# One-hot compares by groups of four chunks, and no unread gather, in a fused attention, expert and gating kernel

## The chip, the cores and the metric

The kernel runs on one core of a Trainium2 chip. The metric is the device time of one execution in microseconds; less is better. Three executions of the kernel before are shown, with one profiled execution among them.

## What is computed

Three layers in a row, all in float32, for 2 batches of 768 tokens with 384 features. First a linear attention with decay, 8 heads of 48. Then a mixture of 8 experts, in which each token goes to one expert, and last a gating layer with a spatial mix. The part around the change is the choice of the expert and the sorting of tokens by expert:

```python
for b in range(B):
    prev_e = -1
    for s in range(S):
        fresh_e = int(np.argmax(logits[b, s]))
        if s == 0 or local_gate[b, s] < 0.5:
            e = fresh_e
        else:
            e = prev_e if prev_e >= 0 else fresh_e
        prev_e = e
        ...
        h = np.maximum(x[b, s] @ w1[e], 0.0)
        out[b, s] = p[e] * (h @ w2[e])
```

The third layer takes relu(x @ w_in), halves it into u and v, normalises v over its features, mixes it over the tokens with w_spatial and a bias, multiplies with u and applies w_out.

## The kernel before, in words

The 1536 tokens are NC = 12 chunks of P = 128, a token on each partition. The kernel has one program for each engine, and the order of the work is written out by hand in each; they meet by semaphores alone. Three stages follow each other, with only weight loads and their splitting running across the borders.

*Attention* (to about 82 us). For each chunk TensorE multiplies, VectorE scales and masks (`mask`, L665, and `decay`, L657), GpSimd makes the bonus products, and ScalarE stores each pair of chunks of x to `x_dram` (`store_rows`, semaphore `s_xd`). Row 0 of `x_dram` is zero, token n is row n + 1. The router's logits of each chunk are made at L1206.

*Routing* (to about 98 us). VectorE computes, in some twenty small steps, `slot_i`: for each token its place in a list sorted by expert, where expert e has room for 1536 places. It is split by bits: `lo_i` (the last seven bits, the place within a block of 128) and `hi_i` (the block). `spread` (L762) is 1 where block `hi_i` is one of 16 blocks, the first two of each expert, and `spread_r` (L767) is `spread` times the token's row number. `place` (L771) is, for each chunk c, a 128 x 128 matrix with a 1 where `lo_i` of the token equals the column number from `iota_w`. The product of `place` and `spread_r`, summed over the twelve chunks in `bank[4]` (L1250), is the list of row numbers: column 2e + t holds the 128 rows that expert e takes in its half t. VectorE copies it to `inv` (L774, semaphore `s_inv`), and GpSimd gathers with it from `x_dram` into `x_in` (`gather_x`, L574, two indirect DMAs for each expert, their semaphores `s_xin`). TensorE transposes what has landed (`transpose_x`, L1264), ScalarE makes the high part `xT_h` (L1033), VectorE the low part `xT_l` (L794), and the first expert matmul (L1256) can start. Between its steps TensorE runs filler matmuls (`stay_warm`, L1129), whose results nobody reads.

The `place` compares are twelve instructions on VectorE, one for each chunk, each with its own step of `s_place`; the twelve matmuls on TensorE each wait for theirs. A compare of that form takes its scalar from a float32 column, which is `lo_f`, a cast of `lo_i` (L761). `Chain.link` makes an engine wait for the instruction it wraps.

GpSimd, after the attention, waits for all rows of x and for the zero row, clears `row_0` (L581), issues an indirect DMA by it (L582) that reads row 0 of `x_dram` 128 times into the tile `one_hot`, and then waits for `s_inv`. Its data is not used; its semaphore `s_unread` is waited for only in the body that handles experts with more than 256 tokens, before `one_hot` is written there.

*Experts and gating.* For each expert 96 matmuls with 256 columns, then 48 with 384; weights arrive as float32 in `raw`, and ScalarE and VectorE split them into a high and a low part (L394, L399). Between the last expert and the gating stage come the tests for overflow blocks, and the gathers of y.

The change also bears on where tiles lie: they are placed one behind the other, in steps of 32 bytes per partition, so tiles behind two that go move down.

Of the kernel before, what the change touches and what calls it, by code (L numbers as in the profile page):

```python
# [9 lines left out]
U32 = mybir.dt.uint32  # L10
ALU = mybir.AluOpType
# [3 lines left out]
P = 128  # L15
B, H, S, DH = 2, 8, 768, 48
D = H * DH
# [4 lines left out]
NC = B * NCB  # L22
# [29 lines left out]
def build(nc, r_feat, k_feat, r_tok, k_tok, v_tok, w_feat, u_tok, w_route, w1, w2, w_in, w_spT, b_sp, w_out, out):  # L52
    x_dram = nc.dram_tensor("x_dram", (NTOK + 1, D), F32).ap()
# [7 lines left out]
    with ExitStack() as ctx:  # L61
        taken = [0]

        def sb(name, shape, dt=F32, scope=ctx):
            size = 2 if dt == BF16 else 4
            for n in shape[1:]:
                size *= n
            taken[0] += -(-size // 32) * 32
            return scope.enter_context(nc.sbuf_tensor(name, shape, dt))

        def sem(name):
            return ctx.enter_context(nc.semaphore(name))
# [18 lines left out]
        iota_w = sb("iota_w", [P, BLK])  # L91
        one_hot = sb("one_hot", [P, 2, BLK])
# [22 lines left out]
        upto = sb("upto", [P, E, NC])  # L115
        row_of = sb("row_of", [P, E, NC])
        lo_i = sb("lo_i", [P, NC], I32)
        lo_f = sb("lo_f", [P, NC])
        row_0 = sb("row_0", [P, 1], U32)
        hi_i = sb("hi_i", [P, NC], I32)  # L120
        col_no = sb("col_no", [P, 2 * E])
        token = sb("token", [P, NC])
# [51 lines left out]
        place = sb("place", [P, NC, P], F32R, scope=att)  # L174
# [111 lines left out]
        s_place = sem("s_place")  # L286
        s_inv_p = sem("s_inv_p")
        s_inv = sem("s_inv")
        s_unread = sem("s_unread")
        s_meta = sem("s_meta")  # L290


# [87 lines left out]
        def raw_as(q, k):  # L380
            return raws[q][:, :].rearrange("p (k m) -> p k m", k=k)
# [111 lines left out]
        def _(pool):  # L493
            chain = Chain(pool, s_pool)
# [27 lines left out]
            for n in range(NC):  # L522
                p, q = divmod(n, 2)
# [48 lines left out]
            def gather_x(e):  # L572
                for t in range(2):
# [3 lines left out]

            pool.wait_ge(s_xd, 16 * NI)
            pool.wait_ge(s_zrow, 32)

            chain.link(nc.gpsimd.memset(row_0[:, :], 0))  # L581
            nc.gpsimd.indirect_dma_start(out=one_hot[:, :, :].rearrange("p a j -> p (a j)")[:, 0:D], out_offset=None,  # L582
                                         in_=x_dram, in_offset=bass.IndirectOffsetOnAxis(ap=row_0[:, 0:1], axis=0))\
                .then_inc(s_unread, 16)
            pool.wait_ge(s_inv, 1)
            gather_x(0)
            for e in range(1, E):
# [34 lines left out]
        def _(dve):  # L622
            chain = Chain(dve, s_dve)
# [101 lines left out]
            def per_e(ap):  # L725
# [32 lines left out]
                                               ALU.max))  # L758
            nc.vector.tensor_scalar(hi_i[:, :], slot_i[:, :], -P, None, ALU.bitwise_and)
            chain.link(nc.vector.tensor_scalar(lo_i[:, :], slot_i[:, :], P - 1, None, ALU.bitwise_and))  # L760
            nc.vector.tensor_copy(lo_f[:, :], lo_i[:, :])  # L761
            chain.link(nc.vector.tensor_tensor(spread[:, :, :],  # L762
                                               hi_i[:, :].rearrange("p (c a) -> p c a", a=1)
                                               .to_broadcast([P, NC, 2 * E]),
# [2 lines left out]
            nc.vector.tensor_tensor(spread_r[:, :, :], spread[:, :, :],  # L767
                                    token[:, :].rearrange("p (c a) -> p c a", a=1).to_broadcast([P, NC, 2 * E]),
                                    ALU.mult)
            for c in range(NC):  # L770
                nc.vector.tensor_scalar(place[:, c, :], iota_w[:, 0:P], lo_f[:, c:c + 1], None, ALU.is_equal)\  # L771
                    .then_inc(s_place, 1)
            dve.wait_ge(s_inv_p, 1)
            nc.vector.tensor_copy(inv[:, :], bank[4][:, 0:2 * E]).then_inc(s_inv, 1)  # L774
            nc.vector.tensor_copy(slot_f[:, :], slot_i[:, :])
# [106 lines left out]
            with dve.If(last >= 1):  # L882
                with dve.Fori(1, NOV + 1) as i:
                    with dve.If(i <= last):
                        dve.wait_ge(o_raw, i * 64)
                        for q, (high, low) in enumerate(((w1_h[:, :, 0:FH], w1_l[:, :, 0:FH]),
                                                         (w1_h[:, :, FH:F], w1_l[:, :, FH:F]),
                                                         (w2_h[:, 0:KF // 2, :], w2_l[:, 0:KF // 2, :]),
                                                         (w2_h[:, KF // 2:KF, :], w2_l[:, KF // 2:KF, :]))):
                            raw = raw_as(q, high.shape[1])  # L890
                            nc.vector.tensor_copy(high, raw).then_inc(o_split, 1)
                            dve.wait_ge(o_split, (i - 1) * 8 + (2 * q + 1))
                            nc.vector.tensor_tensor(low, raw, high.bitcast(F32), ALU.subtract).then_inc(o_split, 1)
                        dve.wait_ge(s_unread, 16)
                        nc.vector.tensor_tensor(rel[:, :], slot_f[:, :], ov_base[:, bass.ds(i - 1, 1)]
                                                .to_broadcast([P, NC]), ALU.subtract).then_inc(o_rel, 1)
                        dve.wait_ge(o_rel, i)
                        for c in range(NC):
                            if c >= 2:
                                dve.wait_ge(o_take, (i - 1) * NC + (c - 1))  # L900
                            nc.vector.tensor_scalar(one_hot[:, c % 2, :], iota_w[:, :], rel[:, c:c + 1], None,
                                                    ALU.is_equal).then_inc(o_hot, 1)
                        dve.wait_ge(o_take, i * NC)
                        for k in range(KD):
                            nc.vector.tensor_copy(xT_h[:, k, :], bank[5 + k][:, 0:BLK]).then_inc(o_xh, 1)
                        dve.wait_ge(o_xh, i * KD)
                        for k in range(KD):
                            nc.vector.tensor_tensor(xT_l[:, k, :], bank[5 + k][:, 0:BLK], xT_h[:, k, :].bitcast(F32),
                                                    ALU.subtract).then_inc(o_xl, 1)
                        for fp in range(4):  # L910
                            k = slice(2 * fp, 2 * fp + 2)
                            high = hT_h[:, k, :].rearrange("p k t -> p (k t)")
                            dve.wait_ge(o_up, (i - 1) * 4 + (fp + 1))
                            nc.vector.tensor_scalar(high, bank[fp][:, :], 0.0, None, ALU.max).then_inc(o_hh, 1)
                            dve.wait_ge(o_hh, (i - 1) * 4 + (fp + 1))
                            nc.vector.scalar_tensor_tensor(hT_l[:, k, :].rearrange("p k t -> p (k t)"), bank[fp][:, :], 0.0,
                                                           high.bitcast(F32), ALU.max, ALU.subtract).then_inc(o_hl, 1)
                        dve.wait_ge(o_yout, i * 32)
                        for t in range(2):
                            dve.wait_ge(o_down, (i - 1) * 2 + (t + 1))  # L920
                            nc.vector.tensor_copy(y_out[:, t, :], bank[4 + t][:, 0:D]).then_inc(o_yev, 1)
# [201 lines left out]
        def _(pe):  # L1123
# [122 lines left out]
            mm(bank[2][:, 0:E * NC], later_b[:, :], hot_v, start=False, stop=True).then_inc(s_count, 1)  # L1246
            stay_warm(11, ident[:, :])
            for c in range(NC):
                pe.wait_ge(s_place, c + 1)
                done = mm(bank[4][:, 0:2 * E], place[:, c, :], spread_r[:, c, :], start=(c == 0), stop=(c == NC - 1))  # L1250
            done.then_inc(s_inv_p, 1)
            pe.wait_ge(s_bbc, 16)
# [202 lines left out]
```

## Time and profile before

| | us |
|---|---|
| three executions | 382.17, 384.67, 390.24 |
| median | 384.67 |
| profiled execution, own time | 384.67 |
| profiled execution, span | 382.9 |
| mean granted TensorE clock, share of full | 0.987 |

The span runs from the first to the last instruction of the profiled execution; its own time holds 1.8 us more around it. Full clock is 2.4 GHz. In the rows, PE is TensorE's matmuls, PEld its weight loads, DVE VectorE, ACT ScalarE, POOL GpSimd, and SPq the queue of the engine that issues most DMAs. L12 is line 12 of the kernel before. `<-` behind an idle time names what ended it.

### The profile page before, as it was taken

How to read it: one execution, taken by the hardware profiler on the slowest of the kernel's cores; microseconds unless marked ns; L12 is line 12 of the kernel's file. 1: busy time of each engine (PE TensorE's matmuls, PEld its weight loads, DVE VectorE, ACT ScalarE, POOL GpSimd, SP SyncE). 2: the span in 40 equal slices, each digit the busy share in tenths (PEclk: the TensorE clock that was granted, in tenths of full speed). 3: DMA queues.
4: the chain of work that ended last, by engine and by line, in shares of the span. 5: the costliest groups of instructions: out<-in, count | busy, mean ns of one | idle time of the engine just before them, and what ended most of it. 6: DMA issues, size and time to landing. Idle time of an engine off the chain costs nothing.

```text
span 382.9 us, 6205 instructions
## 1 busy us (share of the span) xinstructions
PE 364.2 (95%) x2515; PEld 348.8 (91%) x2515; DVE 224.0 (59%) x389; ACT 141.7 (37%) x216; POOL 105.4 (28%) x123
## 2 busy tenths in 40 slices
PE   5899999999799999999999999499999999999996
PEld 5799899986799999999999999278999998899996
DVE  6799689638684958687484955048035605605530
ACT  1023233322364645557272434047411326621122
POOL 2697999612110203031010000515700002500000
PEclk9999999999899999999999999699999999999999
DMA  6989989821595767869594510500310020000002
GB/s 225 409 307 353 388 342 325 300 84 53 166 334 176 237 242 253 299 211 348 182 308 162 184 43 21 145 2 3 89 37 0 0 99 26 2 0 2 0 29 95
DMA packets 30863, 61.97 MB, mean 162 GB/s; under 512 B 2433, under 2 KB 17794, under 8 KB 30834
## 3 DMA queue, kind: packets, MB, share of 16 engines
q1 hardware_dynamic: 23762, 48.00, 35.4%
q10 hardware_dynamic: 5216, 7.87, 5.7%
q0 software_dynamic: 1856, 5.70, 4.8%
q8 instruction: 21, 0.34, 0.4%
q14 instruction: 8, 0.07, 0.1%
HBM read 51.53 MB, written 10.03 MB: 161 GB/s over the span
## 4 chain that ended last, share of the span: by engine, by line
PE 91%; DMA 3%; DVE 2%; issue 2%; SPq 1%; ACT 1%; POOL 0%; DVEq 0%
PE bank L1256 23%; PE bank L1258 23%; PE bank L1257 23%; PE bank L1183 6%; PE bank L1140 3%; PE bank L1179 2%; PE bank L1163 2%; DMA vN<-v_tok 2%; PE bank L1206 2%; PE bank L1153 1%; PE bank L1264 1%; PE bank L1129 1%; PE bank L1196 1%; PE bank L1352 1%; DMA x_in<-x_dram,inv 1%
## 5 line engine op out<-in xcount | busy, mean ns | idle before, releaser
L1256 PE MATMUL bank<-xT_h,w_h 128*128 128x256 f32 x192 | 55.0, 287 | 1.6 <-DVE xT_l L794 1.6
L399 DVE TENSOR_TENSOR w_l<-raw,w_h 128x1536 fp32r<-128x1536 f32 x29 | 50.4, 1758 | 10.2 <-ACT w_h L394 10.2
L1258 PE MATMUL bank<-xT_h,w_l 128*128 128x256 f32 x192 | 55.0, 287 | 0.0
L1257 PE MATMUL bank<-xT_l,w_h 128*128 128x256 f32 x192 | 55.0, 287 | 0.0
L394 ACT ACTIVATE w_h<-raw 128x1536 fp32r<-128x1536 f32 x32 | 46.9, 1485 | 12.3 <-DVE inv L774 8.0
L574 POOL DMA_INDIRECT x_in<-x_dram,inv x16 | 19.0, 1187 | 96.1 <-PE bank L1264 86.8
L1256 PE MATMUL bank<-w_h,hT_h 128*128 128x384 f32 x128 | 43.4, 339 | 0.0
L1258 PE MATMUL bank<-w_h,hT_l 128*128 128x384 f32 x128 | 42.8, 334 | 0.0
L1257 PE MATMUL bank<-w_l,hT_h 128*128 128x384 f32 x128 | 42.8, 334 | 0.0
L1038 ACT ACTIVATE hT_h<-bank 128x512 fp32r<-128x512 f32 x32 | 19.0, 594 | 59.5 <-PE bank L1258 59.5
L1256 PEld LDWEIGHTS bank<-xT_h,w_h 128*128 128x128 f32 x192 | 37.5, 195 | 1.9 <-DVE xT_l L794 1.9
L1258 PEld LDWEIGHTS bank<-xT_h,w_l 128*128 128x128 f32 x192 | 37.6, 196 | 0.0
L1257 PEld LDWEIGHTS bank<-xT_l,w_h 128*128 128x128 f32 x192 | 37.5, 195 | 0.0
L608 POOL TENSOR_TENSOR v_l<-v_nrm,v_h 128x512 fp32r<-128x512 f32 x12 | 15.5, 1292 | 64.9 <-ACT v_h L1096 64.9
L857 DVE SCALAR_TENSOR_TENSOR hT_l<-bank,hT_h 128x512 fp32r<-128x512 f32 x32 | 21.8, 686 | 17.7 <-ACT hT_h L1038 17.7
L1258 PE MATMUL bank<-w_sp_h,v_l 128*128 128x384 f32 x96 | 32.1, 334 | 0.0
L1256 PE MATMUL bank<-w_sp_h,v_h 128*128 128x384 f32 x96 | 32.1, 334 | 0.0
L1257 PE MATMUL bank<-w_sp_l,v_h 128*128 128x384 f32 x96 | 32.1, 334 | 0.0
L959 DVE TENSOR_TENSOR gate_in<-bank,b_bc 128x384 f32<-128x384 f32 x16 | 8.9, 558 | 35.4 <-PE bank L1258 35.4
L1183 PE MATMUL bank<-vN,scores 128*128 128x96 f32 x192 | 28.2, 275 | 0.0
L1183 PEld LDWEIGHTS bank<-vN,scores 128*128 128x128 f32 x192 | 24.8, 192 | 0.0
L1105 ACT ACTIVATE g_h<-gated 128x384 fp32r<-128x384 f32 x16 | 8.4, 527 | 42.9 <-DVE gated L963 42.9
(194 smaller groups left out, 812.3 us busy)
## 6 DMA issues: line engine op xcount, KB each, us to landing
raw<-w SPq DMA_DIRECT2D x28, 768.0 KB
vN<-v_tok SPq DMA_DIRECT2D x6, 576.0 KB, 6.6
rT<-r_feat SPq DMA_DIRECT2D x6, 512.0 KB, 7.2
kT<-k_feat SPq DMA_DIRECT2D x6, 512.0 KB, 8.3
kN<-k_tok SPq DMA_DIRECT2D x6, 512.0 KB, 8.6
raw<-w ACTq DMA_DIRECT2D x4, 768.0 KB
y_dram<-y_out SPq DMA_DIRECT2D x16, 192.0 KB, 1.9
rN<-r_tok SPq DMA_DIRECT2D x6, 384.0 KB, 7.1
```

The costliest lines, as they stand in the source:

```text
L394: nc.scalar.activation(parts[n][3], raw_of(n), ACT.Copy).then_inc(s_high, 1)
L399: eng.tensor_tensor(low, raw_of(n), high.bitcast(F32), ALU.subtract).then_inc(s_low[kind], 1)
L574: nc.gpsimd.indirect_dma_start(out=x_in[:, t, :], out_offset=None, in_=x_dram, in_offset=bass.IndirectOffsetOnAxis(ap=inv[:, 2 * e + t:2 * ...
L608: nc.gpsimd.tensor_tensor(v_l[:, c, :], v_nrm[q][:, :], v_h[:, c, :].bitcast(F32), ALU.subtract).then_inc(g_vl, 1)
L857: nc.vector.scalar_tensor_tensor(hT_l[:, k, :].rearrange("p k t -> p (k t)"), bank[fp][:, :], 0.0, hT_h[:, k, :].rearrange("p k t -> p (k ...
L959: nc.vector.tensor_tensor(gate_in[q][:, :], bank[3 + f][:, 0:HALF], b_bc[:, t * HALF:(t + 1) * HALF], ALU.add).then_inc(g_sin, 1)
L1038: nc.scalar.activation(hT_h[:, 2 * fp:2 * fp + 2, :].rearrange("p k t -> p (k t)"), bank[fp][:, :], ACT.Relu).then_inc(s_hh, 1)
L1140: done = mm(bank[2 * q + head % 2][:, m * CH:(m + 1) * CH], k_dec[q][rows, m, :], r_dec[n % 3][rows, m, :], start=True, stop=True)
L1183: done = mm(bank[4 + q][:, at:at + 2 * DH], scores[q][:, g * NP + m, :], vN[:, p % 2, q, m, g * DH:(g + 2) * DH], start=first_one, stop=Tr ...
L1256: mm(dst, left_h, right_h, start=(k == 0), stop=False)
L1257: mm(dst, left_h, right_l, start=False, stop=False)
L1258: return mm(dst, left_l, right_h, start=False, stop=(k == last_k))
```

## The change

The twelve compares that write `place` become three, each for four chunks, in a form with two tensor inputs: `lo_i` (int32), repeated along the columns, against `iota_w`, repeated along the chunks. Each of the three raises `s_place` by one, and TensorE waits once for each four matmuls. `lo_f` is no longer made. Beside that, the gather into `one_hot` that nobody reads goes, with `row_0`, its semaphore and the wait for it. Two tiles go, of 64 and 32 bytes per partition with rounding.

```diff
--- before.py
+++ after.py
@@ -115,8 +115,6 @@
         upto = sb("upto", [P, E, NC])
         row_of = sb("row_of", [P, E, NC])
         lo_i = sb("lo_i", [P, NC], I32)
-        lo_f = sb("lo_f", [P, NC])
-        row_0 = sb("row_0", [P, 1], U32)
         hi_i = sb("hi_i", [P, NC], I32)
         col_no = sb("col_no", [P, 2 * E])
         token = sb("token", [P, NC])
@@ -286,7 +284,6 @@
         s_place = sem("s_place")
         s_inv_p = sem("s_inv_p")
         s_inv = sem("s_inv")
-        s_unread = sem("s_unread")
         s_meta = sem("s_meta")
 
 
@@ -577,11 +574,6 @@
 
             pool.wait_ge(s_xd, 16 * NI)
             pool.wait_ge(s_zrow, 32)
-
-            chain.link(nc.gpsimd.memset(row_0[:, :], 0))
-            nc.gpsimd.indirect_dma_start(out=one_hot[:, :, :].rearrange("p a j -> p (a j)")[:, 0:D], out_offset=None,
-                                         in_=x_dram, in_offset=bass.IndirectOffsetOnAxis(ap=row_0[:, 0:1], axis=0))\
-                .then_inc(s_unread, 16)
             pool.wait_ge(s_inv, 1)
             gather_x(0)
             for e in range(1, E):
@@ -758,7 +750,6 @@
                                                ALU.max))
             nc.vector.tensor_scalar(hi_i[:, :], slot_i[:, :], -P, None, ALU.bitwise_and)
             chain.link(nc.vector.tensor_scalar(lo_i[:, :], slot_i[:, :], P - 1, None, ALU.bitwise_and))
-            nc.vector.tensor_copy(lo_f[:, :], lo_i[:, :])
             chain.link(nc.vector.tensor_tensor(spread[:, :, :],
                                                hi_i[:, :].rearrange("p (c a) -> p c a", a=1)
                                                .to_broadcast([P, NC, 2 * E]),
@@ -767,9 +758,12 @@
             nc.vector.tensor_tensor(spread_r[:, :, :], spread[:, :, :],
                                     token[:, :].rearrange("p (c a) -> p c a", a=1).to_broadcast([P, NC, 2 * E]),
                                     ALU.mult)
-            for c in range(NC):
-                nc.vector.tensor_scalar(place[:, c, :], iota_w[:, 0:P], lo_f[:, c:c + 1], None, ALU.is_equal)\
-                    .then_inc(s_place, 1)
+            for g in range(3):
+                c = slice(g * NC // 3, (g + 1) * NC // 3)
+                nc.vector.tensor_tensor(place[:, c, :], lo_i[:, c].rearrange("p (c a) -> p c a", a=1)
+                                        .to_broadcast([P, NC // 3, P]),
+                                        iota_w[:, 0:P].rearrange("p (a j) -> p a j", a=1)
+                                        .to_broadcast([P, NC // 3, P]), ALU.is_equal).then_inc(s_place, 1)
             dve.wait_ge(s_inv_p, 1)
             nc.vector.tensor_copy(inv[:, :], bank[4][:, 0:2 * E]).then_inc(s_inv, 1)
             nc.vector.tensor_copy(slot_f[:, :], slot_i[:, :])
@@ -891,7 +885,6 @@
                             nc.vector.tensor_copy(high, raw).then_inc(o_split, 1)
                             dve.wait_ge(o_split, (i - 1) * 8 + (2 * q + 1))
                             nc.vector.tensor_tensor(low, raw, high.bitcast(F32), ALU.subtract).then_inc(o_split, 1)
-                        dve.wait_ge(s_unread, 16)
                         nc.vector.tensor_tensor(rel[:, :], slot_f[:, :], ov_base[:, bass.ds(i - 1, 1)]
                                                 .to_broadcast([P, NC]), ALU.subtract).then_inc(o_rel, 1)
                         dve.wait_ge(o_rel, i)
@@ -1246,7 +1239,8 @@
             mm(bank[2][:, 0:E * NC], later_b[:, :], hot_v, start=False, stop=True).then_inc(s_count, 1)
             stay_warm(11, ident[:, :])
             for c in range(NC):
-                pe.wait_ge(s_place, c + 1)
+                if c % (NC // 3) == 0:
+                    pe.wait_ge(s_place, 3 * c // NC + 1)
                 done = mm(bank[4][:, 0:2 * E], place[:, c, :], spread_r[:, c, :], start=(c == 0), stop=(c == NC - 1))
             done.then_inc(s_inv_p, 1)
             pe.wait_ge(s_bbc, 16)
```

## Rows read from the trace of the kernel before

**Rows 1.** The page: busy time of TensorE; the chain that ended last, by engine.

```profile
PE 364.2 (95%) x2515; PEld 348.8 (91%) x2515; DVE 224.0 (59%) x389; ACT 141.7 (37%) x216; POOL 105.4 (28%) x123
...
PE 91%; DMA 3%; DVE 2%; issue 2%; SPq 1%; ACT 1%; POOL 0%; DVEq 0%
```

**Rows 2.** The chain of waits, 88 to 99 us: start, length, what.

```profile
89.13 2.45 PE bank L1250 x12
...
93.39 3.06 DMA x_in<-x_dram,inv
...
98.69 0.39 PE bank L1256
```

**Rows 3.** Timeline of all engines, 88 to 92 us: start, length, instruction, count.

```profile
88.05 0.17 DVE L761 CAST lo_f<-lo_i 128x12 f32<-128x12 int32 x1
88.13 0.35 DVE L762 TENSOR_TENSOR spread<-hi_i,col_no 128x192 f32<-128x192 int32 x1
...
88.79 2.43 DVE L771 TENSOR_SCALAR place<-iota_w,lo_f 128x128 fp32r<-128x128 f32 x12
89.13 2.34 PEld L1250 LDWEIGHTS bank<-spread_r,place 128*128 128x128 f32 x12 [0.46 <-DVE place L771]
```

**Rows 4.** VectorE by line and shape: count, busy us, mean ns, idle before.

```profile
L665 DVE TENSOR_TENSOR scores<-bank,later 128x512 f32<-128x512 f32 x24 | 15.3, 678 | 0.2 <-PE bank L1140 0.2
L657 DVE TENSOR_TENSOR k_dec<-kT,tab_k 128x512 f32<-128x512 f32 x12 | 11.6, 965 | 0.9 <-DMA kT<-k_feat 0.8
...
L771 DVE TENSOR_SCALAR place<-iota_w,lo_f 128x128 fp32r<-128x128 f32 x12 | 2.4, 279 | 0.0
...
L762 DVE TENSOR_TENSOR spread<-hi_i,col_no 128x192 f32<-128x192 int32 x1 | 0.4, 351 | 0.0
```

**Rows 5.** Timeline of TensorE: the router at 80.8, the first expert at 100 and 104.

```profile
80.83 0.84 PE L1206 MATMUL bank<-w_rt,xT_att 128*128 128x9 f32 x6
...
99.99 0.42 PE L1256 MATMUL bank<-xT_h,w_h 128*128 128x256 f32 x1
100.21 0.41 PE L1257 MATMUL bank<-xT_l,w_h 128*128 128x256 f32 x1
...
104.00 0.28 PE L1257 MATMUL bank<-xT_l,w_h 128*128 128x256 f32 x1
104.12 0.28 PE L1258 MATMUL bank<-xT_h,w_l 128*128 128x256 f32 x1
```

**Rows 6.** Timeline of GpSimd, 83 to 94 us.

```profile
83.98 1.17 POOL L582 DMA_INDIRECT one_hot<-x_dram,row  x1 [0.30 <-POOL row L581]
92.05 1.04 POOL L574 DMA_INDIRECT x_in<-x_dram,inv  x1 [6.89 <-DVE inv L774]
```

**Rows 7.** Lines L574, L946 and L1250: durations in ns, min/median/max.

```profile
L574 POOL DMA_INDIRECT x_in<-x_dram,inv x16: 944/948/2468, 92.0 to 199.3; - x16
...
L946 DVE TENSOR_SCALAR v_nrm<-v_act,mean_var,std x12: 545/578/777, 255.9 to 332.2; 128x512 f32<-128x512 f32 x12
...
L1250 PE MATMUL bank<-spread_r,place x12: 277/277/278, 89.1 to 91.3; 128*128 128x16 f32 x12
```

**Rows 8.** DMA issues: count and us from issue to landing.

```profile
one_hot<-x_dram,row POOLq DMA_INDIRECT x1, 3.9
```

**Rows 9.** Stretches: length, busy us of each engine, granted clock, DMA share, GB/s.

```profile
8.00:12.00 4.00, 1.75 (x20) 1.39 (x20) 3.57 (x7) 0.60 (x1) 1.03 (x2) 1.00 1.03 423
86.00:88.00 2.00, 1.92 (x18) 1.93 (x19) 1.61 (x8) 0.00 (x0) 0.00 (x0) 1.00 0.32 85
96.00:99.00 3.00, 0.86 (x5) 0.62 (x6) 1.39 (x3) 0.87 (x2) 1.37 (x2) 1.00 0.05 9
99.00:104.00 5.00, 5.00 (x31) 5.00 (x30) 3.73 (x3) 1.84 (x2) 0.52 (x1) 0.66 0.68 199
243.00:250.00 7.00, 4.33 (x8) 2.16 (x9) 0.00 (x0) 0.00 (x0) 3.34 (x4) 0.51 0.51 148
```

**Rows 10.** Timeline between the experts and the gating stage.

```profile
245.68 3.78 PE L1129 MATMUL bank<-b_bc,ident 128*128 128x512 f32 x4 [4.97 <-issue]
```

## Prediction

> **What bounds the kernel now.** I read the page first: TensorE is busy in 95% of the span; the chain that ended last runs over it for 91% [rows 1]. The sum can therefore change only where TensorE has nothing useful to do. The edited lines lie in one such place, between the router and the first expert. There the chain of waits, in order of time, is the second view [rows 2]: VectorE builds `lo_i`, `lo_f`, `spread` and `spread_r` one by one, twelve compares write `place`, twelve matmuls at L1250 turn it into the list of rows, VectorE copies that to `inv`, GpSimd issues two gathers, the second one's landing releases the transposes, ScalarE and VectorE split them, and the first expert matmul starts at 98.69; its long pieces are the rows shown. Everything in this chain is serial, so a microsecond here is a microsecond of the span. The reader is to see in [rows 2, 3, 6] that the gathers with their issues (92.05 to 96.45) are longer than the whole piece that is rewritten (88.05 to 91.58).
>
> The profiled execution took 384.67 us, of which 382.9 is the span and 1.8 lies around it; it is also the median of the three runs shown (382.17 to 390.24), so a sum against it is a sum against the median.
>
> **Part 1: `lo_f` goes.** The cast starts at 88.05 and the next instruction already at 88.13 [rows 3]: VectorE lets the following one in 0.08 us later, and the link behind it waited for `spread`, not for the cast. Gain 0.08.
>
> **Part 2: twelve compares become three.** Before, the first `place` starts at 88.79, and twelve take 2.43 us in all at 279 ns each [rows 3, 4]: (2.43 - 0.28)/11 = 0.195 from start to start, an overlap of 0.084. The new form has two tensor inputs and 4x128 = 512 outputs. The row of its size is the mask, 128x512 with a broadcast operand, 678 ns [rows 4]; `spread`, with an int32 input and two broadcasts, lies no higher: 351 ns for 192 elements, so 0.155 + 1.02 ns an element through both rows. GpSimd is idle from 85.15 to 92.05 [rows 6], so the long cases of the same size, `k_dec` at 965 ns, which run beside GpSimd work, are only the upper bound. With the same overlap of 0.084 the three end at 88.71 + 2 x 0.594 + 0.678 = 90.58. Before, the last ends at 88.79 + 2.43 = 91.22. So VectorE is done 0.64 earlier. By the upper bound (965 ns) they would end at 88.71 + 2 x 0.881 + 0.965 = 91.44, 0.22 later than now.
>
> One rule speaks against this step. A one-input operation with per-partition scalars takes at least 545 ns for 512 elements [rows 7], against 279 for 128, which is 0.69 ns for each further element; two-input ones take the 1.02 [rows 4]. The Trainium skill, "VectorE: DVE Perf Modes", section "Mode 2×_2P — use both read ports for one tensor", says that fp32 tensor_scalar may run at two results a cycle while tensor_tensor stays at one. By that rule alone, at 0.96 GHz, the old form would be 12 x 0.067 = 0.80 us of elements and the new 1.60, and the edit would lose 0.80; the trace agrees with its direction, but shows that at 128 elements the fixed part of each instruction is larger than what the rule saves.
>
> **The tail on TensorE.** This is where I choose. Today each matmul at L1250 follows its own compare: the first load starts at 89.13, 0.06 after its compare ended, and the last matmul ends at 91.58, 0.36 after the last compare [rows 2, 3]. After the change four matmuls are released together by the last compare, at 90.58 + 0.06 = 90.64. How fast four 128x128 loads with 16 moving columns follow each other isn't in the trace, because VectorE paces them. Bounds: no faster than all at once; no slower than today's pace, (2.45 - 0.277)/11 = 0.198 [rows 2, 7]. Nearest is the router's matmul, also a 128x128 load with few columns: six in 0.84 us, (0.84 - 0.277)/5 = 0.113 apart if one takes as long [rows 5]. I take it, the more so as the expert's matmuls load a fresh 128x128 every 0.12 us [rows 5]. The last one ends at 90.64 + 0.277 + 3 x 0.113 = 91.26; before, 91.58. Gain of parts 1 and 2 together: 0.32 us. With no time between them it is 91.58 - 90.92 = 0.66, with 0.198 it is 0.07; with the slow 965 ns compares and 0.113 it becomes a loss of 0.54. TensorE's first release moves to 88.71 + 0.678 + 0.06 = 89.45 from 89.13.
>
> **Part 3: the unread gather goes.** The gather takes 1.17 us up to 85.15, and GpSimd then idles 6.89 us until `inv` [rows 6]. Its data moves alone: 85 GB/s in 86 to 88 [rows 9], which is 0.17 MB of its 0.20. So its time costs nothing now and its removal gives nothing. What it may have bought is that the first useful gather isn't the first of its kind. Issue: 1.17 against 1.04 for the next one, and a median of 0.948 for all sixteen [rows 6, 7]: +0.13 on the path if that is a first-use cost. Landing: 3.9 us [rows 8] against 3.06 for the one on the path [rows 2], 0.84 longer. I book only the 0.13: the transposes' split waits for both gathers, the second is issued 1.34 us after the first, so a first landing 0.84 late still lands ahead of the second one. Bounds: -0.13 (the issue at 92.05 gets shorter instead, as the median is by 0.09, plus some rounding) and +0.97 (0.13 + 0.84, if the second is held up too).
>
> **The rest.** The wait on `s_unread` and its users stand in the body for overflow blocks; between the experts and the fillers of the gating stage TensorE sits idle for 4.97 us up to 245.68 [rows 10], so no matmul of that body runs. Nothing gained. The tiles behind `lo_f` and `row_0` move down by 96 bytes. At the start, transfers into them reach 423 GB/s with the 16 DMA engines full [rows 9]; there is little to win by another address. Zero, at most 0.1 us either way. Nine fewer waits of TensorE cost nothing, it waits for the same compares.
>
> Sum: 384.67 - 0.32 + 0.13 = 384.48, say **384.5 us**.
>
> **The rivals.** *A cold gather on the path.* The missing first use shows in the landing of the second gather too: 384.48 + 0.84 = 385.3. For it: the only long landing at a quiet time is the very first. Against: that gather read one row 128 times, which may be slow by itself, and the one on the path took 3.06.
>
> *The clock.* While it waits for the gather, TensorE does 0.86 us of work in 3, and soon after, the granted clock falls: 0.66 on average in 99 to 104 [rows 9], which is 2 x 0.34 x 5 = 3.4 us at 1.2 GHz. Matmuls then start 0.22 apart instead of 0.12 [rows 5], so these 3.4 us hold 15.5 instead of 28.3, a loss of 12.8 x 0.12 = 1.5 us. A shift of some tenths may make the fall vanish: 384.48 - 1.5 = 383.0. The Trainium skill, "TensorE: Matmul & The Clock Gate", section "What's actually happening", says that the gate's watch isn't reset when a kernel starts; by that, one trace can't tell whether the next execution has this fall; no run here shows it yet, and it weighs on both signs.
>
> *Slower than before: the two together.* The first real gather bears all of the first use (+0.97), TensorE idles nearly a microsecond longer before the first expert, and the clock stays at 1.2 GHz for a second stretch as long as the first (+1.5): 384.67 - 0.32 + 0.97 + 1.5 = 386.8. Its place is L574 to L1256 at 92 to 104; it decides once the wait behind the transposes and the split exceeds today's by enough for the fall to come before 98.7. For it: around the 4.97 us gap that ends at 245.68 the clock is at half for 7 us (0.51 in 243 to 250) [rows 9, 10]. Against: the issue cost seen is 0.13 only.
>
> *TensorE was the pace.* The loads of L1250 lie end to end (12 in 2.34 us, [rows 3]) with one recorded idle. If they can't go faster than 0.198, the twelve start at 89.45 and end at 91.90, 0.32 later than now: 384.67 + 0.32 + 0.13 = 385.1. Against: 0.12 at the expert's loads.
>
> **How the numbers follow.** Forecast 0.45; cold gather 0.15; clock fall gone 0.12; both together 0.13; TensorE's pace 0.10; anything outside these 0.05. All terms are far below 2% (7.7 us), about what a measurement of this kernel can tell from no change. The cases reach from 383.0 to 386.8; three executions of one and the same kernel lay 2.5 under and 5.6 over their median, so I add 1.2 below and 0.8 above for the median: 381.8 to 387.6. Over 2% faster has no mechanism (0.01); over 2% slower needs a first-use cost several times what the rows show (0.04); within 2%: 0.95.
>
> **What would show it.** Three `place` rows of about 0.68 us starting near 88.7 to 89.9 on this time scale; L1250 in groups of four, the last ending 0.3 earlier against `spread_r`; the first x_in issue at about 1.17 and the second landing some 3.1 us after its issue; no `one_hot` transfer. The forecast is wrong if the issue or landing of the first gathers grows by over a microsecond, if the compares take near 1 us, or if the stretch at 1.2 GHz is absent or doubled; then the matching rival holds. If none of these shows and the time is off all the same, it comes from a stage that I hold to be untouched.

## The result: 1.2% slower, and the profile after

| | before | changed |
|---|---|---|
| six executions each, median, us | 384.68 | 388.88 |
| lowest and highest, us | 382.17, 390.24 | 387.37, 390.41 |
| ratio, 95% interval | | 1.012 [1.0077, 1.0165] |
| profiled execution: own time, span, us | 384.67, 382.9 | 386.37, 384.6 |
| twelve executions beside 29 of before, later, median, us | 384.65 | 387.06 |
| ratio there, 95% interval | | 1.0063 [1.0027, 1.0099] |

The ratios leave out executions more than 1.5% above the fastest of their kernel; medians and mean clocks are over all, unless said otherwise. The loss is within the 2% that I called no change, but clear of noise. The first median lies outside my range of 381.8 to 387.6, the later one of 387.06 just inside it. Between the two profiled executions the difference is only 1.7 us; the changed kernel's was one of its quicker ones.

The page of the changed kernel shows the same picture as [rows 1], a little lower on TensorE:

```profile
PE 362.9 (94%) x2515; PEld 347.6 (90%) x2515; DVE 224.4 (58%) x379; ACT 141.6 (37%) x216; POOL 105.2 (27%) x121
...
PE 90%; DMA 3%; DVE 2%; issue 2%; SPq 1%; ACT 1%; POOL 0%; DVEq 0%; POOLq 0%
```

The chain of waits, which answers to [rows 2]: start, length, what.

```profile
91.42 0.19 DVE inv L768
...
91.68 0.82 issue
92.50 1.18 POOL x_in L571
...
93.98 3.99 DMA x_in<-x_dram,inv
...
100.20 0.58 PE bank L1250
```

From the start of `inv` to the first expert matmul it was 98.69 - 91.60 = 7.09 us before (`inv` began at 91.60 there) and is 100.20 - 91.42 = 8.78 now. The 1.69 us more are three pieces: the first gather starts 1.08 behind the start of `inv` instead of 0.45 (+0.63; the 0.82 "issue" is time in which GpSimd waited for nothing that the profile shows), it takes 1.18 instead of 1.04 (+0.14), and the second gather lands 3.99 behind its start instead of 3.06 (+0.93).

The timeline of the changed kernel shows the third piece, and the compares; it answers to [rows 3] and [rows 6].

```profile
88.83 1.89 DVE L763 TENSOR_TENSOR place<-lo_i,iota_w 128x512 fp32r<-128x512 int32 x3
...
89.57 1.82 PE L1244 MATMUL bank<-spread_r,place 128*128 128x16 f32 x12 [0.59 <-DVE place L763]
...
92.50 1.18 POOL L571 DMA_INDIRECT x_in<-x_dram,inv  x1 [18.57 <-DVE inv L768]
...
93.22 1.76 DVE L396 TENSOR_TENSOR w_l<-raw,w_h 128x1536 fp32r<-128x1536 f32 x1 [0.30 <-ACT w_h L391]
...
93.98 1.83 POOL L571 DMA_INDIRECT x_in<-x_dram,inv  x1 [0.30 <-issue]
```

The second gather's issue (the time in which GpSimd executes the instruction that starts the transfer) takes 1.83 us, 0.88 more than before. What differs is who was first. Line L396 is VectorE's low part of expert 1's first weights. Before, it and the second gather both started at 93.39. Now it starts at 93.22, the gather at 93.98, and the gather's issue ends at 95.81, 0.83 us after the VectorE instruction has ended at 94.98.

The new compares, which answer to [rows 4]: three, 684 ns each.

```profile
L763 DVE TENSOR_TENSOR place<-lo_i,iota_w 128x512 fp32r<-128x512 int32 x3 | 1.9, 684 | 0.0
```

And the stretches of [rows 9]: no transfer in 86 to 88; the clock falls to the same mean in 99 to 104, now with less work in that stretch, since the first expert starts 1.5 later.

```profile
86.00:88.00 2.00, 1.88 (x18) 1.81 (x18) 1.61 (x8) 0.00 (x0) 0.00 (x0) 1.00 0.00 0
99.00:104.00 5.00, 3.80 (x20) 3.80 (x21) 4.42 (x4) 0.49 (x3) 1.73 (x2) 0.66 0.46 100
243.00:250.00 7.00, 3.05 (x4) 1.41 (x5) 0.00 (x0) 0.00 (x0) 4.42 (x5) 0.76 0.69 193
```

### The profile page after: what moved, and what is told of

Read it like the earlier page. It is cut to its first block, busy times and chain, and to the rows that moved or that the text cites. A ratio compares the mean times of both kernels' runs of the same rounds, so it can differ in the third digit from the quotient of the medians.

```text
span 384.6 us, 6193 instructions
## 1 busy us (share of the span) xinstructions
PE 362.9 (94%) x2515; PEld 347.6 (90%) x2515; DVE 224.4 (58%) x379; ACT 141.6 (37%) x216; POOL 105.2 (27%) x121
## 4 chain that ended last, share of the span: by engine, by line
PE 90%; DMA 3%; DVE 2%; issue 2%; SPq 1%; ACT 1%; POOL 0%; DVEq 0%; POOLq 0%
PE bank L1250 23%; PE bank L1252 23%; PE bank L1251 23%; PE bank L1176 6%; PE bank L1133 3%; PE bank L1172 2%; PE bank L1156 2%; DMA vN<-v_tok 2%; PE bank L1199 2%; PE bank L1146 1%; PE bank L1258 1%; PE bank L1189 1%; PE bank L1122 1%; DMA x_in<-x_dram,inv 1%; PE bank L1346 1%
## 5 line engine op out<-in xcount | busy, mean ns | idle before, releaser
L1250 PE MATMUL bank<-xT_h,w_h 128*128 128x256 f32 x192 | 55.1, 287 | 1.6 <-DVE xT_l L788 1.6
L396 DVE TENSOR_TENSOR w_l<-raw,w_h 128x1536 fp32r<-128x1536 f32 x29 | 50.4, 1756 | 9.8 <-ACT w_h L391 9.0
L571 POOL DMA_INDIRECT x_in<-x_dram,inv x16 | 19.8, 1237 | 107.9 <-PE bank L1258 86.9
L1250 PE MATMUL bank<-w_h,hT_h 128*128 128x384 f32 x128 | 43.4, 339 | 0.0
L1250 PEld LDWEIGHTS bank<-xT_h,w_h 128*128 128x128 f32 x192 | 37.4, 195 | 1.9 <-DVE xT_l L788 1.9
L1250 PE MATMUL bank<-w_sp_h,v_h 128*128 128x384 f32 x96 | 32.1, 334 | 0.0
```

Source lines behind the costliest of these rows:

```text
L396: eng.tensor_tensor(low, raw_of(n), high.bitcast(F32), ALU.subtract).then_inc(s_low[kind], 1)
L571: nc.gpsimd.indirect_dma_start(out=x_in[:, t, :], out_offset=None, in_=x_dram, in_offset=bass.IndirectOffsetOnAxis(ap=inv[:, 2 * e + t:2 * ...
L1250: mm(dst, left_h, right_h, start=(k == 0), stop=False)
```

## The experiments

The question was which of the three edits costs, and then what stands behind each of the three pieces. No kernel leaves out a part of the computation. "Behind `inv`" is counted from the start of the copy to `inv`, unless I say from its end (0.17 to 0.19 us later), as my expectations did.

**compares_only.** The changed kernel with the gather put back (here and below, the tile, the semaphore and the wait for it in the overflow body come back with it, and are not shown):

```diff
             pool.wait_ge(s_zrow, 32)
+            chain.link(nc.gpsimd.memset(row_0[:, :], 0))
+            nc.gpsimd.indirect_dma_start(out=one_hot[:, :, :].rearrange("p a j -> p (a j)")[:, 0:D], out_offset=None,
+                                         in_=x_dram, in_offset=bass.IndirectOffsetOnAxis(ap=row_0[:, 0:1], axis=0))\
+                .then_inc(s_unread, 16)
             pool.wait_ge(s_inv, 1)
```

> The changed kernel with the unread gather put back: only the compares differ from the kernel before (and 64 bytes of tiles). Theory (the removed gather is what costs): ratio to before at or just under 1, 0.998 to 1.001, some 0.3 us faster, first expert matmul about 7.1 us after inv. Rival (the compares, or their gap on TensorE, cost): ratio 1.008 to 1.016 as in the changed kernel.

Measured: ratio 0.9988 [0.9947, 1.0029]. Its timeline: the first gather 0.45 behind `inv`, the second not held up though VectorE's instruction started 0.02 earlier, first expert matmul 7.16 behind `inv`. Neither the compares nor TensorE's wider gap ahead of the first `place` cost anything that this comparison, good to 0.4%, can see.

```profile
86.08 1.21 POOL L581 DMA_INDIRECT one_hot<-x_dram,row  x1 [0.30 <-POOL row L580]
...
96.74 0.17 DVE L775 CAST inv<-bank 128x16 uint32<-128x16 f32 x1 [1.72 <-PE bank L1252]
...
97.19 1.05 POOL L573 DMA_INDIRECT x_in<-x_dram,inv  x1 [9.90 <-DVE inv L775]
...
98.53 1.81 DVE L398 TENSOR_TENSOR w_l<-raw,w_h 128x1536 fp32r<-128x1536 f32 x1 [0.30 <-ACT w_h L393]
98.55 0.95 POOL L573 DMA_INDIRECT x_in<-x_dram,inv  x1 [0.31 <-issue]
...
103.90 0.38 PE L1258 MATMUL bank<-xT_h,w_h 128*128 128x256 f32 x1 [1.64 <-DVE xT_l L795]
```

**gather_gone_only.** The kernel before, with its twelve compares and all tiles in place, without the gather:

```diff
-            chain.link(nc.gpsimd.memset(row_0[:, :], 0))
-            nc.gpsimd.indirect_dma_start(out=one_hot[:, :, :].rearrange("p a j -> p (a j)")[:, 0:D], out_offset=None,
-                                         in_=x_dram, in_offset=bass.IndirectOffsetOnAxis(ap=row_0[:, 0:1], axis=0))\
-                .then_inc(s_unread, 16)
...
-                        dve.wait_ge(s_unread, 16)
```

> The kernel before without the unread gather, tiles left where they are: the twelve compares stay. Theory: ratio 1.008 to 1.016, first x_in issue over 0.8 us after inv, the second issue near 1.8 us, landing near 4.0, first expert matmul 8.5 to 9 us after inv. Rival (compares or tile addresses): ratio 0.998 to 1.003.

Measured: 1.0074 [1.0034, 1.0113], just under the expected range. The whole pattern is back: 1.08, 1.18, 1.83, and 8.66 to the first expert matmul. The removed gather is the loss; the tiles' addresses aren't.

```profile
91.53 0.17 DVE L770 CAST inv<-bank 128x16 uint32<-128x16 f32 x1 [0.37 <-PE bank L1245]
...
92.61 1.18 POOL L574 DMA_INDIRECT x_in<-x_dram,inv  x1 [18.86 <-DVE inv L770]
...
93.33 1.76 DVE L399 TENSOR_TENSOR w_l<-raw,w_h 128x1536 fp32r<-128x1536 f32 x1 [0.30 <-ACT w_h L394]
...
94.09 1.83 POOL L574 DMA_INDIRECT x_in<-x_dram,inv  x1 [0.30 <-issue]
...
100.19 0.57 PE L1251 MATMUL bank<-xT_h,w_h 128*128 128x256 f32 x1 [1.64 <-DVE xT_l L790]
```

**gather_early.** The changed kernel with an unread gather of rows of `w_out` among the attention work:

```diff
+                if n == 2:
+                    chain.link(nc.gpsimd.memset(row_0[:, :], 0))
+                    nc.gpsimd.indirect_dma_start(..., in_=w_out, ...).then_inc(s_unread, 16)
```

> The changed kernel with a gather that nobody reads put among GpSimd's attention work at about 20 us (rows of w_out, by a zero index), some 70 us of other GpSimd work and waiting ahead of the first useful one. If the cost is a first use alone (code or rings made ready once), it is gone: ratio 0.997 to 1.003, first x_in issue 0.3 us after inv. If it is the pause or the other work since the last gather, it stays: ratio 1.007 to 1.016, and first matmul 8.5 us or more after inv.

Measured in only six executions: 1.0199 [1.0111, 1.0288], an interval that lies on both sides of 2%, and worse than either expectation. Why it is that much isn't shown. Its profile has `inv` at 94.16, but the changed kernel itself has it at 91.42 in one execution and at 94.59 in another (changed_again), so that says nothing of the edit. The time as a whole can't be read for the question; the timeline of GpSimd can:

```profile
30.86 1.17 POOL L573 DMA_INDIRECT one_hot<-w_out,row  x1 [0.30 <-POOL row L572]
...
95.13 0.98 POOL L580 DMA_INDIRECT x_in<-x_dram,inv  x1 [18.53 <-DVE inv L777]
96.42 2.11 POOL L580 DMA_INDIRECT x_in<-x_dram,inv  x1 [0.30 <-issue]
```

The first useful gather still starts 0.97 behind `inv`, so a first use long ago doesn't cure the late start. But its own length is 0.98, not 1.18, and now the early one has the 1.17: 0.2 us belong to the first gather of a program, whenever it comes.

**plain_dma_warm.** A plain DMA in the gather's place:

```diff
+            nc.gpsimd.dma_start(one_hot[:, :, :].rearrange("p a j -> p (a j)")[:, 0:D], x_dram[1:P + 1, :])\
+                .then_inc(s_unread, 16)
             pool.wait_ge(s_inv, 1)
```

> The changed kernel with a plain GpSimd DMA of 128 rows of x_dram in the place of the unread gather. If GpSimd's DMA queue or rings must be made ready, this does it too: ratio 0.997 to 1.003. If it is the indirect instruction's own code, nothing is won: ratio 1.007 to 1.016 and the issue of the first x_in gather as late as in the changed kernel (0.9 us after inv). In between: landing back to 3.1 us, but the late issue stays, some 0.7 us of the 1.7.

Measured: 1.0049 [1.001, 1.0088], between the two.

```profile
83.35 0.79 POOL L580 DMA_DIRECT2D one_hot<-x_dram  x1 [9.49 <-DMA x_dram<-X]
...
91.36 0.18 DVE L773 CAST inv<-bank 128x16 uint32<-128x16 f32 x1 [0.70 <-PE bank L1250]
...
91.83 1.12 POOL L573 DMA_INDIRECT x_in<-x_dram,inv  x1 [7.69 <-DVE inv L773]
...
93.15 1.76 DVE L398 TENSOR_TENSOR w_l<-raw,w_h 128x1536 fp32r<-128x1536 f32 x1 [0.30 <-ACT w_h L393]
93.25 2.49 POOL L573 DMA_INDIRECT x_in<-x_dram,inv  x1 [0.30 <-issue]
```

The first gather starts 0.47 behind `inv`: the late start is cured, and not by an indirect DMA. Yet the first expert matmul comes 9.00 behind `inv`, later than in the changed kernel, because the second gather starts only 0.10 us behind VectorE's instruction and is held for 2.49 us, to 0.83 after its end (94.91). My "in between" case had the parts the wrong way round: start cured, landing not.

**low_after_move.** The changed kernel, one order changed on VectorE:

```diff
-            make_low(dve, first[1])
             move_x(0)
+            make_low(dve, first[1])
```

> The changed kernel with one order changed on VectorE: the low part of expert 1's first weights (make_low of first[1]) comes behind the move of x for expert 0, not ahead of it. Theory (the second gather's issue is held up by the VectorE instruction that started 0.8 us before it, a port that both need): the second issue falls from 1.83 to 0.95 us, its landing stays near 3.0 us behind its start, the first expert matmul comes 0.9 us earlier after inv (8.78 to 7.9), ratio 1.002 to 1.008, some 0.9 us under the changed kernel. Rival (the second issue is long because GpSimd's code or rings are cold): it stays at 1.8 and the time stays or rises.

Measured: 1.001 [0.9972, 1.0047]. The second issue is 0.96 us, the first expert matmul 7.92 behind `inv` instead of 8.78, as expected, while the late start (1.07) and the 1.18 stay. The ratio is a little better than the 1.002 to 1.008 that I had expected. The moved instruction now meets the first gather for expert 2, whose issue takes 2.25 us at 111.99; the ratio holds whatever that costs.

```profile
94.24 0.17 DVE L768 CAST inv<-bank 128x16 uint32<-128x16 f32 x1 [0.70 <-PE bank L1244]
...
95.31 1.18 POOL L571 DMA_INDIRECT x_in<-x_dram,inv  x1 [19.51 <-DVE inv L768]
...
96.80 0.96 POOL L571 DMA_INDIRECT x_in<-x_dram,inv  x1 [0.30 <-issue]
...
102.16 0.39 PE L1250 MATMUL bank<-xT_h,w_h 128*128 128x256 f32 x1 [1.71 <-DVE xT_l L788]
```

Over all kernels of this study the second gather's issue reads:

| kernel | VectorE's start ahead of the second gather's | its issue | ends after VectorE's end |
|---|---|---|---|
| before | 0.00 | 0.95 | not held |
| compares_only | 0.02 | 0.95 | not held |
| kept_filled | 0.01 | 0.95 | not held |
| plain_dma_warm | 0.10 | 2.49 | 0.83 |
| gather_before_wait | 0.45 | 2.12 | 0.81 |
| gather_early | 0.47 | 2.11 | 0.82 |
| changed, memset_in_place, fill_the_wait, gather_gone_only, changed_again | 0.74 to 0.76 | 1.82 to 1.85 | 0.82 to 0.83 |

The Trainium skill, "SBUF — State Buffer", section "SBUF: two separate sides", says that VectorE and GpSimd share a port pair, and that a VectorE operation with two SBUF inputs contends for it with a GpSimd operation that reads SBUF: whichever starts first has it for the whole instruction, and the other is blocked. The table agrees: a gather that is later by 0.10 us or more waits to the end. What it shows beyond this is that an indirect DMA's issue behaves like such an operation, and ends some 0.8 us behind the release.

Other places in the traces sharpen it. The three long issues further on in the kernel before fit too; the longest is the first pair of rows. A short instruction with two SBUF inputs does the same: `hit` (L782), 0.32 us long, started 0.11 ahead of the first useful gather of [rows 6], which ended 0.83 behind its end. So the 1.04 there is an issue of 0.95 with a short hold in it. The last pair is the counter-case: `hT_l` reads one of its inputs from PSUM (the tile `bank`), and a gather that starts within it isn't held.

```profile
146.38 1.76 DVE L399 TENSOR_TENSOR w_in_l<-raw,w_in_h 128x1536 fp32r<-128x1536 f32 x1 [1.16 <-ACT w_in_h L394]
146.49 2.47 POOL L574 DMA_INDIRECT x_in<-x_dram,inv  x1 [0.30 <-issue]
...
91.94 0.32 DVE L782 TENSOR_TENSOR hit<-expd,hot 128x96 f32<-128x96 f32 x1
...
162.49 0.68 DVE L857 SCALAR_TENSOR_TENSOR hT_l<-bank,hT_h 128x512 fp32r<-128x512 f32 x1
162.85 0.95 POOL L574 DMA_INDIRECT x_in<-x_dram,inv  x1 [13.89 <-PE bank L1264]
```

Over the 14 traces together, 61 gathers started 0.07 us or more behind a VectorE split of weights (L399 before), and all 61 ended 0.82 to 0.83 behind its end; 14 started 0.00 to 0.03 behind one, and none was held. Of 113 that started within an `hT_l` or `xT_l`, both with an input in PSUM, none took over 0.95.

**memset_in_place.** Only the memset where the gather was.

```diff
             pool.wait_ge(s_zrow, 32)
+            chain.link(nc.gpsimd.memset(row_0[:, :], 0))
             pool.wait_ge(s_inv, 1)
```

> The changed kernel with only the 128x1 memset where the unread gather was. If the late start of the first gather (0.89 us after inv, 0.29 before) comes from GpSimd having executed nothing for 18 us, a memset at 83.6 us cures it as any instruction would: start 0.3 us after inv. If it comes from the DMA-issuing code not having been used lately: start stays 0.85 to 0.95 us after inv. The issue stays at 1.18 and the second at 1.8 either way.

Measured in a single execution: 388.07 us, and in the timeline the start is 1.05 behind `inv` (0.88 from its end). Executing something isn't enough.

```profile
84.92 0.10 POOL L580 MEMSET row<- 128x1 uint32 x1 [9.64 <-DMA x_dram<-X]
...
92.81 0.17 DVE L772 CAST inv<-bank 128x16 uint32<-128x16 f32 x1 [0.70 <-PE bank L1248]
...
93.86 1.18 POOL L573 DMA_INDIRECT x_in<-x_dram,inv  x1 [8.84 <-DVE inv L772]
```

**gather_before_wait.** The unread gather (of `w_out`) ahead of the wait for the rows of x:

```diff
+            chain.link(nc.gpsimd.memset(row_0[:, :], 0))
+            nc.gpsimd.indirect_dma_start(..., in_=w_out, ...).then_inc(s_unread, 16)
             pool.wait_ge(s_xd, 16 * NI)
```

> The changed kernel with an unread gather (of w_out, by a zero index) as GpSimd's next work behind its last attention product, at about 74 us, ahead of its wait for the rows of x; then GpSimd idles some 17 us. If the late start of the first useful gather comes from other work having been done in between (as behind the early gather at 30 us), it is cured here: start 0.45 us after inv has begun, as before, issue 1.04. If it is the length of the idle time, it stays at 0.9 to 1.1. The second issue is 0.95 or about 2.4 in the first case, by whether it meets the VectorE instruction, and 1.8 in the second.

Measured in a single execution: 388.04 us.

```profile
76.71 1.18 POOL L579 DMA_INDIRECT one_hot<-w_out,row  x1 [0.30 <-POOL row L578]
...
93.57 0.17 DVE L775 CAST inv<-bank 128x16 uint32<-128x16 f32 x1 [0.70 <-PE bank L1252]
...
94.55 0.96 POOL L573 DMA_INDIRECT x_in<-x_dram,inv  x1 [16.66 <-DVE inv L775]
...
95.36 1.76 DVE L398 TENSOR_TENSOR w_l<-raw,w_h 128x1536 fp32r<-128x1536 f32 x1 [0.30 <-ACT w_h L393]
...
95.81 2.12 POOL L573 DMA_INDIRECT x_in<-x_dram,inv  x1 [0.30 <-issue]
```

No other work lies between this gather and the useful one, only 16.66 us of idle time, and the start is late, 0.98 behind `inv`. The second issue isn't the 1.8 that I expected with a late start: the first gather starts 0.10 earlier than in the changed kernel and its issue is 0.2 shorter, so the second starts only 0.45 behind VectorE and takes 2.12. In compares_only 9.90 us of idle time lay between the two and the start was 0.45.

So an earlier DMA issue of GpSimd cures the late start where a memset doesn't, but not from here. Idle time by itself does no harm up to 15.4 us. In the kernel before, the gather for expert 3 waits 15.41 us for the transposes and starts 0.27 behind their end at 127.35. The first gather of that kernel starts 0.28 behind the end of `inv`, that of the changed kernel 0.90.

```profile
126.53 0.82 PE L1264 MATMUL bank<-ident,x_in 128*128 128x128 f32 x6
...
127.62 1.74 POOL L574 DMA_INDIRECT x_in<-x_dram,inv  x1 [15.41 <-PE bank L1264]
```

If it is idle time, the effect is lost between 15.4 and 16.7 us. If it is what GpSimd's program has between the two gathers (here the waits for x and the zero row, there one wait), it has no such edge. No run separates these two.

**fill_the_wait.** The changed kernel with filler matmuls:

```diff
+            stay_warm(1, b_bc[:, 0:256])
...
+                    if e == 0 and t == 0:
+                        stay_warm(3, b_bc[:, 0:256])
                 done.then_inc(s_xt, 1)
+                if e == 0:
+                    stay_warm(3, b_bc[:, 0:256])
```

> The changed kernel with filler matmuls (128x256) in TensorE's waits for the gathers and for the split: one before the first landing, three between the two landings, three behind the transposes. They write a bank that nobody reads. Theory (part of the loss, 1 us or more, is the clock that falls because the wait has grown): granted clock stays at full through 100 to 104, mean clock of the runs up by some 0.004, ratio 1.001 to 1.007. Rival (the loss is the delay alone): ratio stays 1.008 to 1.012 or rises, as the fillers can only be in the way.

Measured: 1.0047 [1.001, 1.0084], first expert matmul 8.75 behind `inv`. The clock is at full in 99 to 104 (first row), but that doesn't show the fillers at work. In this execution `inv` starts only at 94.92, and the clock had fallen before it, to 0.79 in 82 to 98. The changed kernel without fillers has the same pattern in the profile of changed_again (second and third row):

```profile
99.00:104.00 5.00, 4.02 (x20) 3.01 (x21) 1.41 (x3) 0.87 (x2) 1.69 (x3) 1.00 0.17 44
...
82.00:98.00 16.00, 15.28 (x86) 11.65 (x86) 9.76 (x35) 4.16 (x7) 2.03 (x2) 0.79 0.11 32
...
99.00:104.00 5.00, 2.38 (x14) 1.42 (x13) 1.79 (x3) 0.87 (x2) 1.77 (x2) 1.00 0.22 55
```

The mean clock of its twelve executions is 0.9851. Changed_again's is 0.9828, but 0.9855 without its two longest. So no gain of the clock is shown, and the intervals of 1.0047 and 1.0063 overlap.

**all_kept_and_filled.** Compares, gather kept, low part behind the move, fillers.

```diff
+            nc.gpsimd.indirect_dma_start(...).then_inc(s_unread, 16)
...
-            make_low(dve, first[1])
             move_x(0)
+            make_low(dve, first[1])
...
+                    if e == 0 and t == 0:
+                        stay_warm(1, b_bc[:, 0:256])
                 done.then_inc(s_xt, 1)
+                if e == 0:
+                    stay_warm(3, b_bc[:, 0:256])
```

> The three new compares, the unread gather kept, the low part behind the move of x, and fillers in TensorE's waits (one between the landings, three behind the transposes). Should beat both kernels if the theories hold: second issue never held up, no fall of the clock in 99 to 104: ratio 0.989 to 0.997. If the low part of expert 1's weights comes too late for the loads behind it, or the fall comes from elsewhere, ratio 0.998 to 1.003.

Measured: 1.0011 [0.9972, 1.0051], first expert matmul 7.23 behind `inv`. It doesn't beat the kernel before, a miss of the first expectation.

**kept_low_after_move** is compares_only with the two VectorE lines exchanged as above:

```diff
-            make_low(dve, first[1])
             move_x(0)
+            make_low(dve, first[1])
```

> Three new compares, unread gather kept, low part of expert 1's weights behind the move of x; no fillers. If the issue of the second gather sometimes loses its race in the kernel before too, this gains 0.3 to 1 us over compares_only and is the fastest: ratio 0.993 to 0.998. If it never does, ratio as compares_only, 0.998 to 1.001.

Measured: 0.9996 [0.9947, 1.0045], 7.13 to the first expert matmul. With the gather kept the race isn't lost often enough to be seen.

**kept_filled** is compares_only with one filler between the landings and three behind the transposes:

```diff
+                    if e == 0 and t == 0:
+                        stay_warm(1, b_bc[:, 0:256])
                 done.then_inc(s_xt, 1)
+                if e == 0:
+                    stay_warm(3, b_bc[:, 0:256])
```

> Three new compares, unread gather kept, fillers in TensorE's waits (one of 256 columns between the landings, wait, three behind the transposes), VectorE's order as before. If the fillers keep the clock up where it falls in the kernel before, mean clock of the runs above that of compares_only and ratio 0.990 to 0.997; if the falls lie elsewhere (attention, gating), as the mean clock of the filled kernels so far suggests, ratio 0.998 to 1.002.

Measured: 0.9991 [0.9955, 1.0028]. The fall in 99 to 104 is gone here, with no earlier one in its place, but the one around the gating stage is there (second row), as the rival had it. Nothing beyond noise is won.

```profile
99.00:104.00 5.00, 5.00 (x44) 5.00 (x44) 4.48 (x4) 2.57 (x3) 0.32 (x1) 1.00 0.70 215
243.00:250.00 7.00, 5.14 (x15) 2.86 (x16) 1.02 (x2) 0.87 (x2) 2.04 (x3) 0.76 0.37 111
```

**changed_again.** The changed kernel, unedited.

> The changed kernel as it stands, timed beside the same runs of the kernel before as its repairs. Theory: ratio 1.006 to 1.013; no run with a mean clock of 0.995 or more, where the kernel before has some.

Measured: 1.0063 [1.0027, 1.0099], and none of its 12 executions had a mean clock of 0.994 or more, nor any of the 23 recorded with the first result; of 87 executions of the kernel before, 15 had.

## Why the prediction was wrong

*The place and the chain* were right: all that moved lies between `lo_i` and the first expert matmul.

*Parts 1 and 2* were right in sign and size. Three compares of 684 ns take 1.89 us, where I had 1.87; the last matmul at L1244 ends 0.67 behind the last compare (91.39 against 90.72), where my pace of 0.113 gave 0.68. From the start of `lo_i` to that of `inv` it was 91.60 - 87.85 = 3.75 and is 91.42 - 87.96 = 3.46: a gain of 0.29 for 0.32. The rule on tensor_scalar did not decide, the rival of TensorE's pace fell.

*Part 3 is the step that failed*: "+0.13 on the path", with the argument that "a first landing 0.84 late still lands ahead of the second one". It costs 1.69 us. Three things were missing. First, I looked for the price of a cold gather in the cold gather's own rows [rows 6, 8], its length and its landing. Even the length was set against a row that wasn't clean, the 1.04 with the hold by `hit` in it: an unheld later issue takes 0.95, a first one 1.18. The late start of 0.63 can't stand in those rows: in the kernel before, the unread gather started behind a memset with an idle time of 0.30, like any other. Second, I let a delay of the first gather be swallowed by the order of the two, and didn't ask what the second one would then meet. It was free only because it started in the same hundredth of a microsecond as VectorE's L399. Three gathers of the kernel before had a long issue for this reason, up to 2.47 us: that maximum stands in [rows 7] in the very row from which I took the median, and I passed it by. Third, the two add on the path, though the first is issued 1.3 us ahead.

So the chain loses 1.69 - 0.29 = 1.40 us, where I had forecast a gain of 0.2. gather_gone_only shows this part alone, low_after_move takes back the held issue, plain_dma_warm the late start.

*The rival "the two together"* was the nearest, 386.8: a cold gather and more time at a low clock. Its first term, 0.97, was too small for the same reason. Of its second term this is shown: the measured differences, 2.4 (later) and 4.2 us (first), are larger than the 1.4 of the chain, and the mean clock is lower, 0.980 over the 23 executions of the first session and 0.983 over the later 12, against 0.986 over 87 of the kernel before. And a mean clock of 0.994 or more was reached by none of the 79 executions of kernels whose profile has the first expert matmul 8.66 us or more behind `inv`, but by 30 of the 147 of those that have it at 7.92 or less. So the longer wait goes with more time at the low clock. Low_after_move fits: with only 0.86 us less in the chain it is level with the kernel before.

Why it does is not shown. In the two profiled executions of before and after the stretch at 99 to 104 is alike (0.66 both), the one at 243 to 250 even better after (0.76 for 0.51). In all seven profiles without fillers in which the clock was full from 82 to 97, it fell around the first expert, in six with a long wait and in that of before with a short one. In five others it had fallen in 82 to 98 already, and only kept_low_after_move fell again at the first expert. With fillers and no earlier fall (two profiles) there was none, and yet fill_the_wait, with the long wait filled, never reached 0.994 in 12 executions.

*The range* took its upper end from that rival and 0.8 us; a first-use cost bounded by one warm execution of the same instruction isn't a bound.

## What to carry to other kernels

A transfer or instruction whose result nobody reads may be a warm-up, and its price isn't in its own row: it is the difference between the next useful one with it and without it, which the trace of before can't show. Before removing one, ask what the next user would meet, and how near in time it runs to an engine that shares a port with it. Where a row's median and maximum differ by more than a factor of two, as 948 and 2468 ns here, find out what the long ones have in common, and take the price of an instruction from rows that nothing held; and if two engines race for a port at a known place, put the one that isn't urgent behind the one that is.

## What the runs showed of the hardware

- An issue of an indirect DMA on GpSimd that starts 0.07 us or more behind a VectorE tensor_tensor of 1536 fp32 elements with both inputs in SBUF isn't finished until 0.81 to 0.83 us after that has ended, 61 of 61 times. At 0.00 to 0.03 us behind, 14 of 14 times, it goes through in 0.95, and VectorE's instruction is the longer one by 0.03 to 0.06 (1.79 to 1.82 for 1.76). Within a VectorE instruction with one input in PSUM, 113 of 113 took no more than 0.95.
- The first useful gather starts 0.97 to 1.08 us behind the start of `inv` where GpSimd has issued no DMA before, issued one some 63 us back, or issued one 16.7 us and two more waits back. With an issue 6.8 to 9.9 us back it is 0.45 to 0.47. A plain DMA serves as well as an indirect one, a memset doesn't, and between gathers of the expert loop 15.4 us of idle time do no harm.
- The first gather of a program takes 1.17 to 1.21 us (1.12 behind a plain DMA), later ones that nothing holds up 0.94 to 0.98, however long ago the first was.
